# Attention units of 64 steps and four batches in two half-unit pipelines, in a fused attention and two-MLP kernel

## The reference

```python
B, H, S, D = 4, 8, 768, 48
for t in range(S):                        # attention, a scan over steps, per batch and head
    cur = einsum('bhd,bhe->bhde', u * k[t], v[t])
    y[t] = einsum('bhd,bhde->bhe', r[t], state + cur)
    state = w[t][..., None] * state + einsum('bhd,bhe->bhde', k[t], v[t])
x = y.transpose(0, 2, 1, 3).reshape(B * S, H * D)         # 3072 tokens x 384
h = x @ w_in                                              # 384 -> 1024
solu = h * softmax(h)
x = (solu - mean) / sqrt(var + 1e-6) * g_ln @ w_out       # 1024 -> 384
x = relu(x @ w2_in) ** 2 @ w2_out                         # 384 -> 2048 -> 384
```

## Time and profile before

| | |
|---|---|
| median of 3 runs | 891.85 us (890.92 to 892.67) |
| profiled execution, first to last instruction | 889.9 us |
| what the median has beside that span | 1.95 us |
| PE busy | 804.8 us, 90% of the span |
| DVE, ACT, POOL busy | 527.3, 427.7, 181.4 us |
| share of PE in the chain that ended last | 73% |

### The profile page before, as it was taken

How to read it: one execution, slowest core, us unless ns; L and a number is a source line. 1 busy time by engine, 2 the same in 40 slices (tenths; PEclk the granted TensorE clock), 3 DMA queues, 4 the chain that set the end, 5 groups by cost and what they waited for, 6 DMA issues and landing times.

```text
span 889.9 us, 23575 instructions
## 1 busy us (share of the span) xinstructions
PE 804.8 (90%) x9648; PEld 667.1 (75%) x9648; DVE 527.3 (59%) x906; ACT 427.7 (48%) x716; POOL 181.4 (20%) x189
## 2 busy tenths in 40 slices
PE   2365958999999999999999999899999999999998
PEld 2254848779779779779778778678878778887786
DVE  5657384783883883683783683584584674453333
ACT  4536354673573573473473473363463573342332
POOL 5223222221221221221221221132132131000000
PEclk9978887999999999999999999899999999999999
DMA  5140345147535434334434434344434432333653
GB/s 179 36 124 3 91 162 120 49 145 180 189 127 170 165 123 127 128 126 127 152 112 130 140 111 125 109 144 136 131 108 133 138 140 90 123 127 107 235 190 106
DMA packets 33971, 114.75 MB, mean 129 GB/s; under 512 B 5840, under 2 KB 14544, under 8 KB 33872
## 3 DMA queue, kind: packets, MB, share of 16 engines
q1 hardware_dynamic: 33872, 113.27, 40.7%
HBM read 91.23 MB, written 17.30 MB: 122 GB/s over the span
## 4 chain that ended last, share of the span: by engine, by line
PE 73%; DVE 12%; issue 6%; ACT 4%; POOL 1%; SPq 1%; DMA 1%; DVEq 0%; ACTq 0%; POOLq 0%
PE hid L492 20%; PE acc L505 17%; PE flex L476 12%; PE flex L445 10%; PE flex L375 3%; PE flex L413 3%; PE flex L416 3%; PE flex L459 2%; DVE r_t L618 2%; DVE att L600 2%; DVE solu L659 2%; PE flex L427 1%; ACT att L815 1%; DVE ln_lo L687 1%; DVE w_up L627 1%
## 5 line engine op out<-in xcount | busy, mean ns | idle before, releaser
L492 PE MATMUL hid<-y_hi,w 128*128 128x512 f32 x576 | 198.8, 399 | 3.2 <-DVE y_lo L694 3.2
L505 PE MATMUL acc<-g_hi,w 128*128 128x512 f32 x576 | 197.2, 396 | 1.4 <-DVE g_lo L703 0.9
L815 ACT ACTIVATE r_diag<-r_t 64x512 f32<-64x512 f32 (+1 forms) x168 | 116.6, 694 | 105.8 <-DVE r_t L618 89.7
L699 DVE TENSOR_TENSOR act<-act 128x512 f32<-128x512 f32 x96 | 73.6, 766 | 125.3 <-ACT g_hi L815 125.3
L1010 POOL TENSOR_TENSOR k_t<-k_t,w_up 128x512 f32<-128x512 f32 x72 | 87.4, 1213 | 220.5 <-PE flex L375 160.6
L492 PEld LDWEIGHTS hid<-y_hi,w 128*128 128x128 f32 x576 | 109.0, 189 | 27.2 <-issue 3.6
L505 PEld LDWEIGHTS acc<-g_hi,w 128*128 128x128 f32 x576 | 108.1, 188 | 26.6 <-issue 2.8
L815 ACT ACTIVATE act<-hid 128x512 f32<-128x512 f32 x96 | 57.3, 597 | 135.1 <-PE hid L492 134.9
L492 PE MATMUL hid<-y_lo,w 128*128 128x512 f32 x288 | 113.3, 393 | 0.0
L505 PE MATMUL acc<-g_lo,w 128*128 128x512 f32 x288 | 112.6, 391 | 0.0
L476 PE MATMUL flex<-ln_hi,out_hi 128*128 128x256 f32 x288 | 82.8, 288 | 0.0
(11 more groups left out here) (98 smaller groups left out, 1348.5 us busy)
## 6 DMA issues: line engine op xcount, KB each, us to landing
w<-split_w SPq DMA_DIRECT2D x80, 768.0 KB, 4.4
split_w<-w SPq DMA_DIRECT2D x16, 768.0 KB, 4.1
r_t<-in_rT SPq DMA_DIRECT2D x24, 192.0 KB, 4.9
k_t<-in_kT SPq DMA_DIRECT2D x24, 192.0 KB, 4.7
w_t<-in_wT SPq DMA_DIRECT2D x24, 192.0 KB, 5.6
v_n<-in_vN SPq DMA_DIRECT2D x12, 384.0 KB, 3.3
out<-o_stage SPq DMA_DIRECT2D x5, 768.0 KB, 4.1
x_pack<-x_t SPq DMA_DIRECT2D x72, 48.0 KB, 2.4
```

Source lines behind the costliest of these rows:

```text
L492: last = mm(hid[:, :], w2[:, j % RING, w, k * P:(k + 1) * P], y[:, k, :], start=n == 0, stop=n == len(terms) - 1)
L505: last = mm(acc[:, d], w2[:, j % RING, w, rows], gx[:, j % 2], start=j == 0 and n == 0, stop=j == J2 - 1 and n == 2, skip_group_check=True)
L699: e.tensor_tensor(act[:, j % 2], act[:, j % 2], act[:, j % 2], ALU.mult).then_inc(g_ready, 1)
L815: return nc.scalar.activation(out_, in_, func, **more)
```

## The change

A unit becomes 64 steps of all four batches: `Q = 16` column blocks of 64 steps, still 1024 columns, still 12 units and 256 tokens each. The level tree has six levels, at steps 0, 2, 3, 4, 6, 7. Each level is issued in two halves `h` of eight blocks, with semaphores of their own, and the level's output stays 128x32 tiles. The bonus stands in the same step as level 0. `r` is loaded twice, to `r_t` and straight into `r_pair`, so that level 0 needs no copy by ACT; `k`, `w` and `r` come as full 128-partition tensors with zero rows. `decay_state` moves from the step after the output to step 1 and writes a second state buffer. `output` does all products with the state first, then all products with `v_n` on 64 rows. The features of one head pair are moved by six DMAs of 16 rows, and the rows of `w_in` are put in that order on the host. The gain is folded into the split of `w_out`. The hardware loop is written out.

```diff
-T = 128
-LEVELS = 7
+T = 64
+LEVELS = 6
...
-LEVEL_AT = {1: 0, 3: 1, 4: 2, 6: 3, 7: 4, 8: 5, 9: 6}
+LEVEL_AT = {0: 0, 2: 1, 3: 2, 4: 3, 6: 4, 7: 5}
...
-REPACK = []
...
+REPACK = [(i, k) for i in range(2) for k in range(KD)]
...
+            def load_w_pair(u):
...
+                for i in range(2):
+                    sp.dma_start(r_pair[half_rows(i), i, :], rT[u, half_rows(i)]).then_inc(rp_in, 16)
...
-                for p, src, n, tile, dst in REPACK:
-                    sp.dma_start(x_pack[dst:dst + n, tile, :],
-                                 x_t[src:src + n, p * TOK:(p + 1) * TOK]).then_inc(packed, 16)
+                for i, k in REPACK:
+                    src = HALF * i + k * (HALF - D)
+                    sp.dma_start(x_t[HALF * i + D:HALF * (i + 1), k, :],
+                                 x_t[src:src + HALF - D, KD, :]).then_inc(packed, 16)
...
+            def level(u, l, h):
+
+                pe.wait_ge(right_ready, half_count(u, l - 1, h, LEVELS - 1))
+                pe.wait_ge(k_ready, half_count(u, l - 1, h))
+                pe.wait_ge(level_taken, scores_taken(u, l - 1, h))
...
+                for q in range(Q):
+                    x, b2 = q // 2, q % 2
+                    for i in range(2):
+                        mm(flex[half_rows(i), b2, x * T:(x + 1) * T], state[u % 2][:, q, i], r_t[:, q * T:(q + 1) * T],
+                           start=x == 0, stop=False, skip_group_check=True)
+                pe.wait_ge(vn_in, (u + 1) * 16)
+                for q in range(Q):
+                    x, b2 = q // 2, q % 2
+                    rows = half_rows(b2)
+                    for i in range(2):
+                        last = mm(flex[HALF * i:HALF * i + D, b2, x * T:(x + 1) * T], v_n[rows, x % NBH, head_cols(x, i)],
+                                  att[rows, x, i], start=False, stop=x == NX - 1, skip_group_check=True)
...
-            with pe.Fori(1, NC - 2) as m:
+            for m in range(1, NC - 2):
...
             def attention(u, g, i):
-                if i in CARRY_AT:
-                    carry(u, CARRY_AT[i])
...
+                if i in LEVEL_AT:
+                    l = LEVEL_AT[i]
+                    if l == 0:
+                        carry(u, 0, 0)
+                        carry(u, 0, 1)
+                        w_products(u)
+                    for h in range(2):
+                        if l < IN_BK:
+                            pair_scores(u, l, h)
+                            carry(u, l + 1, h)
...
+            def decay_state(u):
+                pool.wait_ge(w_ready, (u + 1) * LEVELS)
+                pool.wait_ge(k_ready, half_count(u, 0, 1))
```

More of the change, by code:

```diff
@@ L92, in build @@
         out_hi, out_lo = sb("out_hi", [P, J1, DM], F32R), sb("out_lo", [P, J1, DM], F32R)
-        state = sb("state", [P, G, Q, 2, HALF])
+        state = [sb(f"state{n}", [P, Q, 2, HALF]) for n in range(2)]
         u_rows = sb("u_rows", [P, NP])
@@ L290, in attention @@
                     if more:
-                        load_v(u + 1)
+                        load_r(u + 1)
+                elif i == 13 and more:
+                    load_v(u + 1)
             for turn in range(3):
@@ L512, in attention @@
             def attention(u, g, i):
-                if i == 0:
-                    bonus(u)
-                elif i in LEVEL_AT:
-                    level(u, LEVEL_AT[i])
-                elif i == 10:
+                if i in LEVEL_AT:
+                    for h in range(2):
+                        if LEVEL_AT[i] == 0:
+                            level_bonus(u, h)
+                        else:
+                            level(u, LEVEL_AT[i], h)
+                elif i == 9:
                     k_natural(u)
                 elif i == 11:
-                    output(u, g)
-                elif i == 12:
+                    output(u)
+                elif i == 12 and u < NU - 1:
                     state_step(u)
@@ new lines, in pair_scores, with w_products @@
+                e.copy_predicated(dst, keep, src).then_inc(level_taken, 1)
+            def w_products(u):
+                v.wait_ge(w_in, (u + 1) * 16)
+                wait(v, k_ready, u * LEVELS * 2)
+                wait(v, state_decayed, u * 2)
+                for l in range(LEVELS):
+                    w_pair = w_level(l).rearrange("p (a two) -> p a two", two=2)
+                    wait(v, w_ready, u * LEVELS + l)
+                    e.tensor_tensor(w_level(l + 1), w_pair[:, :, 0], w_pair[:, :, 1], ALU.mult).then_inc(w_ready, 1)
@@ L801, in _ @@
             block_turns(0)
-            with v.Fori(1, NC - 2) as m:
+            for m in range(1, NC - 2):
                 block_turns(m)
@@ new lines, in place, with take_level5 @@
+            def place(u, h):
+                xs = slice(HX * h, HX * (h + 1))
+                s.wait_ge(level_taken, scores_taken(u, IN_BK - 1, h))
+                for b2 in range(2):
+                    rows = block_rows(2 * b2)
+                    a(att[rows, xs, :, 0:BK].rearrange("p x i t -> p (x i) t"),
+                      att[rows, xs, :, BK:T].rearrange("p x i t -> p (x i) t"), ACT.Copy).then_inc(placed, 1)
+            def take_level5(u, h):
+                s.wait_ge(level_mm, half_count(u, LEVELS - 1, h))
+                s.wait_ge(placed, u * 4 + 2 * h + 2)
+                for c in range(NBK):
+                    dst = att[block_rows(c % 2 * 2), HX * h:HX * (h + 1), :, BK:T]\
+                        .rearrange("p (b two) i t -> p b two i t", two=2)[:, :, c // 2]
+                    last = a(dst, flex[block_rows(c), h, FCOL:FCOL + P].rearrange("p (b i t) -> p b i t", i=2, t=BK), ACT.Copy)
+                last.then_inc(att_ready, 1)
@@ L861, in x_high, with take_output @@
+            def take_k(u):
+                for h in range(2):
+                    s.wait_ge(knat_mm, u * 2 + h + 1)
+                    a(uk[:, half(h)], flex[:, h], ACT.Copy).then_inc(knat_ready, 1)
+            def take_output(u):
+                wait(s, xlo_ready, u)
+                s.wait_ge(y_mm, u + 1)
+                a(x_t[:, :, 0:HALF * 2], flex[:, 0].rearrange("p (a n) -> p a n", a=NP), ACT.Copy).then_inc(x_ready, 1)
             def x_high(u):
@@ L979, in _ @@
             block_turns(0)
-            with s.Fori(1, NC - 2) as m:
+            for m in range(1, NC - 2):
                 block_turns(m)
```

548 lines of the change are left out of this document (256 added, 292 removed).

## The result

The changed kernel takes **918.77 us** (912.79 to 919.46), the kernel before in the same series 891.38 us (889.92 to 892.67): a ratio of 1.0294, 95% interval 1.0262 to 1.0326. It is slower by 27 us where 34 less were forecast.

The account below looks back on a forecast made before the run. PE's own work and few stops were taken to bound the long stage, chains over several engines turns 0 to 2. 891.85 - 12 - 2 - 7.5 + 5 - 4.5 - 3 - 10 = 857.9, said as 858 us; range 845 to 881.

Parts of the forecast that it names:

- Turn 0, -12: First turn: half-unit levels about 3.1 us apart and fewer repacking transfers start the first MLP earlier; -12 us.
- Loop and half clock at its jump, -4.5 and -3: Long stage: without loop jumps, waits before the bonus go, -4.5 us, and the half-clock stretch at the second jump, -3.
- PE's work, -10: Long stage, nine turns with attention: level 6 gone, output and state step about equal; -10 us, or +11.
- four abreast: Output and state step on PE: 64-row products lie side by side, two by rows and two by columns; 1.2 and 1.1 us.
- Rivals 1 and 3: PE: 64-row products not four side by side, 879 us, chance 0.2; halved-column output records no cheaper, 897 us, chance 0.07.
- rival 3: PE's output: a record gets no cheaper when its columns are halved; slower than before, 897 us, chance 0.07.
- rule of independent tiles: PE's 64-row products: different tiles load weights and multiply in parallel, so the lower bound holds, 1.2 and 1.1 us.
- Turns 1 and 2, -2: Second and third turns: softmax about 2 us later, but 1 to 2 us gained before `narrow1`; -2 us for both.
- Rival 2: First turns: half-unit pipelines do not shorten them, DVE and POOL slow each other, small instructions lose fixed time; 871 us, chance 0.15.
- Waits for the normalised half, -7.5: Long stage: PE's 8.4 us of waits arise from level 6's copies on DVE; without them 7.5 us go.
- New stops, +5: Long stage: near coincidences, such as ACT's copies ahead of squares, stop PE 0.5 us in each of ten turns; +5 us.
- what would make it wrong: New wait of several us each turn: step 2 (level 0 scores), step 4 (ACT's copies) or step 9 (level 5 copies).

Follow-up runs that it names:

- level1_late: Changed kernel with the levels at steps 0, 3, 4, 5, 6, 7 instead of 0, 2, 3, 4, 6, 7; 927.09 us.
- sq_right3: Changed kernel with ACT's squares ahead of level 5's copies, block placing at step 6, and level 3's right-half copies at step 2; 882.08 us.
- sq_right3_decay_both: sq_right3 with POOL's state decay back at step 10 and DVE's run of six decay products cut in two; 867.56 us.
- all_norm_first: sq_right3_decay_both with DVE's normalise of the second token half at step 8, ahead of ln_low; 850.66 us.
- before_place7: Kernel before with ACT's placing of the 32x32 blocks at step 7, ahead of squares, instead of step 9; 919.31 us.
- right3_early: Changed kernel with ACT's right-half copies for level 3 moved from step 3 to step 2, ahead of the exponentials; 897.77 us.
- sq_right3_whole: sq_right3 with ACT's right halves copied in two instructions of 512 columns per level instead of four of 256; 884.29 us.
- sq_right3_decay10b: sq_right3 with POOL's decay of the state back at step 10, where the kernel before has it; 870.39 us.

## Why the prediction was wrong

By its own steps:

- **Turn 0, -12**: right, -10.3; `hidden1` starts at 50.0, forecast 48.3.
- **Loop and half clock at its jump, -4.5 and -3**: right in size, 8.6 to 9.9 us when written out alone. But "the half-clock stretch, which stands right at the second jump, goes with it" took the jump for its only cause: the changed kernel has no jump and eight such stretches, behind other stops.
- **PE's work, -10**: right in sign, and more: -16 over the stage. Of the 6 us more, about 4 are the products with the state, 2.08 us a turn where 2.5 was taken, over nine turns; the rest is not traced. The products on 64 rows take what the forecast took for four abreast:

```profile
420.89 2.08 PE L407 MATMUL flex<-r_t,state 128*64 128x64 f32 x64
422.91 1.11 PE L414 MATMUL flex<-att,v_n 64*48 64x64 f32 x64
428.95 1.15 PE L425 MATMUL flex<-v_n,uk 64*64 64x48 f32 x64
```

  17 ns per record for L414 and 18 for L425, against 33 for L407 on 128 rows. Rivals 1 and 3 are out, though rival 3's 897 us lies nearer to the result than the forecast: what made the kernel slower was another thing. By the rule of independent tiles, which the prediction took from the Trainium skill (TensorEngine Tiling (Array Packing), Key Properties), the trace agrees.
- **Turns 1 and 2, -2**: wrong, +14. The step that failed was "the softmax of the first token half is about 2 us later than now". In turn 1 of the changed kernel `row_max` starts 11.9 us behind the first `hidden1`, before the change 6.0 us:

```profile
61.84 1.22 DVE L644 TENSOR_REDUCE stats<-flex 128x1 f32<-128x1024 f32 x1 [1.79 <-PE flex L443]
```

  I had counted DVE's run and not what PE does meanwhile: it stands in front of level 1 twice (1.67 and 1.25 us), and in the second half of `hidden1` its records take 0.63 us up to 60.3 and 0.40 behind that. The granted clock is 0.75 in the mean of the turn, has 0.86. That the stops lowered it is likely, but not shown apart. How much of the 14 us the late softmax makes is not shown apart: level1_late takes 4.9 of the 5.9 us away and the two turns together lose 3.2, but PE's waits before the levels grow there by 4.2. What shortened the turns: ACT's orders, 5 us of the 14 (sq_right3); decay and products together, 5 (sq_right3_decay_both). The place of `normalise` gives 9 more, which the kernel before might gain as well. So about 4 of the 14 us have no cause shown. Rival 2 had DVE and POOL slow each other; that is so, but it had turn 0 gain only 5 us, and it gained 10.3.
- **Waits for the normalised half, -7.5**: wrong. The step said that these waits "arise because the copies of level 6 stand ahead of L674 to L679 on DVE". With those copies gone the wait is 9.2 us in sq_right3. From the mean (L664 before the change, L654 now) to `normalise` (L674, now L664) it took 6.1 us before the change (388.79 to 394.85 in one turn) and still 5.5 in sq_right3_decay_both: the 1.4 us of DVE's copies were gone, but ACT had eight copies of level 5 in front of `ln_high` instead of four, and `ln_low`, queued ahead of `normalise`, waits for `ln_high`. PE for its part came earlier. all_norm_first shows the cause: with `normalise` ahead of `ln_low` the wait is gone.
- **New stops, +5**: the step at which the forecast turned over. It read ACT's placing and level-5 copies as "about 3.8 us instead of 1.5, behind which `squares` and `ln_high` are queued; they have about 3 us". The copies take 3.96 us, as said. But they have no slack: `squares` is due when the mean is, and in the kernel before it starts 0.04 us behind it (388.97). In before_place7 it starts 1.8 to 3.5 us late in all turns but the last, and the kernel is 28 us slower. I compared its start to `gate`'s end in steps of the list, not in times of the trace. Measured: 14.2 us more waiting for the normalised half, 10.6 for ACT's right halves at step 4 (which I named as a place to look, and priced at nothing), and 12 us more lost to the clock.

For stops and clock in the long stage the forecast had -7.5 + 5 - 4.5 - 3 = -10 us; they came to +28 and +12. Of the places named under "what would make it wrong", step 4 was one. The copies of level 5 were another, though not at step 9, where PE waits 0.4 us for them, but through `squares` and `ln_high` behind them. Put together: the gains forecast for turn 0, the loop and PE's work add up to 12 + 7.5 + 10, measured 10 + 9 + 16. With the stops mended one by one the time goes to 850.66 us. That it is near the 858 forecast does not bear the forecast out, since it takes edits that the forecast did not have. What stays open: the last 4 us of turns 1 and 2; the 9.1 us of PE's idle time there that still end at `gate` (L649) in all_norm_first, as 9.2 us did before the change; and what PE waits for in the stops without a releaser.

## What to carry to other kernels

In hand-ordered queues, price a reordering by slack read in the trace: for each instruction newly queued ahead of another, take the time at which the later one's input is ready, and count every us behind it as a stop of the bound engine until a row shows a gap there. Then follow the late instruction to the next queues, since the stop may come out elsewhere than where it was made (`squares` late, `k` transposes waiting). And where the busy engine has little idle time, stops also cost through the clock (here 12 us on 28 us of added stops), so that mends can give more than their own waits.

## What was not expected of the hardware

- PE at 1.2 GHz while fully busy (207.90 to 211.30, behind 3.44 us of stop). All eight stretches of the changed kernel's long stage, of 3.4 or 6.8 us, begin within 1.3 us of the end of a stop of 1.66 to 3.45 us; five more stops of 1.54 to 2.35 us have none behind them. In sq_right3 even stops of 2.31, 2.31 and 3.26 us have none. So a single stop's price can't be foretold from these rows.
- The loop cost the kernel before 8.6 to 9.9 us. 4.5 are the waits before the bonus and 3.4 the half-clock stretch. Written out, its waits for the normalised half also fell by half (8.4 to 4.3 us); why stays open. Straight code is not free of such waits: right3_early, sq_right3 and sq_right3_whole each have one of 3.3 us in the middle of a level (L381), with nothing that PE waits for.
- DVE's half carry took 1.08 us beside POOL's state decay and 0.45 alone. The half scores, which read PSUM, took 0.43 us both with and without POOL in that stretch, and 0.28 later in the turn. The difference goes with the level and not with POOL: in each unit of sq_right3, sq_right3_decay10b and all_norm_first the four of levels 0 and 1 take 0.42 to 0.46 us, and the six of levels 2 to 4 take 0.28 to 0.30.
